# A decayed attention before two MLP blocks: the chunk of 128 with a carried state and plain float32 scores in two row halves, in place of one split at 256 and three-term scores

## The chip, the cores and the metric

One NeuronCore of a Trainium2 chip runs the whole program. The metric is the device time in microseconds (us) of one execution, the median of several. TensorE (PE) multiplies, VectorE (DVE) and ScalarE (ACT) read PSUM and do elementwise work, SyncE (SP) and GpSimd (POOL) issue the transfers (DMAs).

## What is computed

```python
batch, n_heads, seq, head_dim = (8, 8, 576, 64)
scores = scale * np.matmul(q, k.transpose(0, 1, 3, 2))
gamma = 1.0 - 2.0 ** (-5.0 - np.arange(H))
Dmat = np.where(rel >= 0, gamma[:, None, None] ** rel[None, :, :], 0.0)   # rel = query - key
x = np.matmul(scores * Dmat, v)                                 # no softmax
# tokens = batch * seq = 4608, 8 heads * 64 = 512 columns
h = np.maximum(np.maximum(x @ w1, x @ w2), x @ w3)              # 512 -> 768
x2 = h @ w_out                                                  # 768 -> 512
out = ((x2 @ u1) * (x2 @ u2)) @ u3 @ u_out                      # 512 -> 1024 -> 512
```

Since there is no softmax, a block of keys far behind its queries can be summed first into a 64x64 matrix per head (keys times decayed values, "the state"), which the decayed queries then multiply.

## The kernel before

The program has three phases. In the first, batch 0's attention runs beside the product u3 @ u_out ("wc", eight blocks, `wc_block`), whose weights and those of the first MLP arrive and are split meanwhile. In the second, a loop over b = 1 to 7, PE does the first MLP of batch b - 1 (18 `b_pair`s of two `b_unit`s each, then 8 `c_unit`s; every unit is 12 or 18 matmuls of 288 columns) and the attention of batch b in between. Last come the first MLP of batch 7 and nine tiles of the second MLP.

The MLP products are in float32r, with operands split into a high and a low part and three products (`product`, L725 to L727). Each engine executes its instructions in the order in which they are written; the semaphores between them are counted up. The order within a batch is set by `PAIR_FROM`: before head s come the b_pairs `PAIR_FROM[s]` to `PAIR_FROM[s+1]`, then on PE `values` of the earlier head pair (even s) or `sum_state` (odd s), then `scores` of head s.

For a head pair the attention is:

- `scores`, once per head (L739, L740): five blocks of the causal triangle, each as two float32r products. Rows 0 to 63 of `kstack` hold the keys' high part and rows 64 to 127 their low part, so ACT (`split_head`, L366, L367) and DVE (L548) first split keys and queries.
- DVE multiplies the scores by the decay table (`decay_head`, L566), five instructions per head.
- `sum_state` (L752): two plain float32 matmuls over the first 256 keys, of 128 columns; ACT copies the result (`read_state`, L377).
- `values` (L768, L774): the state times the decayed queries of positions 256 to 575 (128x320), and per key block and head one plain float32 matmul of 64 output rows, head 0 into PSUM partitions 0 to 63 and head 1 into 64 to 127.

A plain float32 matmul shows in the trace as two MATMUL records, each with a weight load (LDWEIGHTS, engine row PEld).

In the wc phase DVE's order matters: `split_u3(s + 1)`, which makes the low part of the next wc block's weights (u3lo), stands behind the attention work of step s. SP's queue loads every head's and pair's arrays, with waits for their buffers; POOL's queue loads u_out, u3 and the MLP weights.

Of the kernel before, what the change touches and what calls it, by code (L numbers as in the profile page):

```python
# [4 lines left out]
P = 128  # L23
# [8 lines left out]
PAIRS = HEADS // 2  # L32
# [5 lines left out]


SPLIT = 256  # L40
REST = SEQ - SPLIT
SB = SPLIT // P
KB = 5

BLOCKS = [
    (0, 0, 0, SPLIT),
    (0, 256, 3, SEQ - 3 * P),
    (0, 448, 4, SEQ - 4 * P),
    (1, 0, 1, SPLIT - P),
    (1, 128, 2, REST),  # L50
]
BANKS = 2
P_AT = [0, 256, 384, 704, 896]
P_COLS = 960
# [5 lines left out]
C_UNITS = KT * 2  # L60
# [4 lines left out]
PAIR_FROM = [0, 3, 5, 7, 9, 11, 13, 15, 18]  # L65
# [5 lines left out]

# [3 lines left out]
def build(nc, qT, kT, kP, vP, w1, w2, w3, w_out, u1, u2, u3T, u_out, decay, qdecay, vdecay, out):  # L75
# [7 lines left out]
    with ctx:  # L83
# [24 lines left out]
        qraw = at("qraw", [P, 2, SEQ], f32, o); o += 2 * SEQ * 4  # L108
        kraw = at("kraw", [P, 2, SEQ], f32, o); o += 2 * SEQ * 4
        qhi = at("qhi", [P, SEQ], f32r, o); o += SEQ * 4  # L110
        qlo = at("qlo", [P, SEQ], f32r, o); o += SEQ * 4
        kstack = at("kstack", [P, SEQ], f32r, o); o += SEQ * 4
        vals = at("vals", [P, 2, KB, P], f32, o); o += 2 * KB * P * 4
        probs = at("probs", [P, 2, P_COLS], f32, o); o += 2 * P_COLS * 4
        dec = at("dec", [P, 2, REST], f32, o); o += 2 * REST * 4
        kblk = at("kblk", [P, SB, P], f32, o); o += SB * P * 4
        vdec = at("vdec", [P, SB, P], f32, o); o += SB * P * 4
        state = at("state", [P, P], f32, o); o += P * 4
        qpair = at("qpair", [P, REST], f32, o); o += REST * 4
        qtab = at("qtab", [P, PAIRS, REST], f32, o); o += PAIRS * REST * 4  # L120
        vtab = at("vtab", [P, HEADS, SB], f32, o); o += HEADS * SB * 4
# [41 lines left out]
        ps_score, ps_state, ps_att, ps_moe = ps[0:2], ps[2], ps[4:6], ps[6:8]  # L163
# [6 lines left out]
        qk_loaded = [sem(f"qk_loaded{i}") for i in range(2)]  # L170
        dec_loaded = [sem(f"dec_loaded{i}") for i in range(2)]
        v_loaded = [sem(f"v_loaded{i}") for i in range(2)]
        split_hi = sem("split_hi")
        split_lo = sem("split_lo")
        scored = sem("scored")
        decayed = sem("decayed")
        vtab_loaded = sem("vtab_loaded")
        qtab_loaded = sem("qtab_loaded")
        k_loaded = sem("k_loaded")
        q_loaded = sem("q_loaded")  # L180
# [3 lines left out]
        state_read = sem("state_read")  # L184
# [50 lines left out]
        def _(sp):  # L235
            def load_head(b, s):
                n = HEADS * b + s
                if not (isinstance(b, int) and n < 2):
                    sp.wait_ge(split_lo, 2 * n - 2)
                for half in range(2):  # L240
                    rows = slice(DH * half, DH * half + DH)
                    sp.dma_start(kraw[rows, s % 2, :], kT[b, s, :, :]).then_inc(qk_loaded[s % 2], 16)  # L242
                for half in range(2):
                    rows = slice(DH * half, DH * half + DH)
                    sp.dma_start(qraw[rows, s % 2, :], qT[b, s, :, :]).then_inc(qk_loaded[s % 2], 16)  # L245
                if not (isinstance(b, int) and n < 2):
                    sp.wait_ge(decayed, BANKS * (n - 1))
                sp.dma_start(dec[:, s % 2, :], decay[s, :, :]).then_inc(dec_loaded[s % 2], 16)

            def load_values(b, p):  # L250
                n = PAIRS * b + p
                if isinstance(b, int) and n < 1:
                    sp.wait_ge(zeroed, 4)
                if not (isinstance(b, int) and n < 2):
                    sp.wait_ge(valued, n - 1)
                sp.dma_start(vals[:, p % 2, 0:4, :],
                             vP[b, p, 0:4 * P, :].rearrange("(n p) c -> p n c", p=P)
                             ).then_inc(v_loaded[p % 2], 16)
                sp.dma_start(vals[0:SEQ - 4 * P, p % 2, 4, :], vP[b, p, 4 * P:SEQ, :]
                             ).then_inc(v_loaded[p % 2], 16)  # L260

                if not (isinstance(b, int) and n < 1):
                    sp.wait_ge(summed, n)
                sp.dma_start(kblk[:, :, :], kP[b, p, 0:SPLIT, :].rearrange("(n p) c -> p n c", p=P)
                             ).then_inc(k_loaded, 16)

            def load_pair_queries(b, p):
                n = PAIRS * b + p
                if not (isinstance(b, int) and n < 1):
                    sp.wait_ge(valued, n)  # L270
                sp.dma_start(qpair[:, :], qT[b, 2 * p:2 * p + 2, :, SPLIT:SEQ].rearrange("h d n -> (h d) n")
                             ).then_inc(q_loaded, 16)

            def load_batch(b):
                for s in range(HEADS):
                    load_head(b, s)
                    if isinstance(b, int) and s == 0:
                        sp.dma_start(vtab[:, :, :], vdecay).then_inc(vtab_loaded, 16)
                    if isinstance(b, int) and s == 1:
                        sp.dma_start(qtab[:, :, :], qdecay).then_inc(qtab_loaded, 16)  # L280
                    if s % 2 == 0:
                        load_values(b, s // 2)
                    else:
                        load_pair_queries(b, s // 2)

            load_batch(0)
            with sp.Fori(1, BATCH) as b:
                load_batch(b)
# [55 lines left out]

# [15 lines left out]
        def _(act):  # L360
            def split_head(b, s):
                n = HEADS * b + s
                act.wait_ge(qk_loaded[s % 2], 64 * (HEADS // 2 * b + s // 2 + 1))
                if not (isinstance(b, int) and n == 0):
                    act.wait_ge(scored, BANKS * n)
                nc.scalar.copy(kstack[:, :], kraw[:, s % 2, :]).then_inc(split_hi, 1)  # L366
                nc.scalar.copy(qhi[:, :], qraw[:, s % 2, :]).then_inc(split_hi, 1)  # L367

            def read_state(b, p):

                n = PAIRS * b + p
                act.wait_ge(summed, n + 1)
                if not (isinstance(b, int) and n == 0):
                    act.wait_ge(valued, n)
                for h in range(2):
                    own = slice(h * DH, h * DH + DH)
                    nc.scalar.copy(state[own, own], ps_state[own, own]).then_inc(state_read, 1)  # L377

            def read_values(b, p):
                n = PAIRS * b + p  # L380
                act.wait_ge(valued, n + 1)
                if not (isinstance(b, int) and b == 0):
                    act.wait_ge(x_lo, n - KT + 1)
                nc.scalar.copy(xraw[:, p, 0:SPLIT], ps_att[0][:, 0:SPLIT]).then_inc(x_out, 1)
                nc.scalar.copy(xraw[:, p, SPLIT:SEQ], ps_att[1][:, 0:REST]).then_inc(x_out, 1)

# [30 lines left out]
            def batch(b):  # L417

                for s in range(HEADS):
                    split_head(b, s)  # L420
                    for i in range(PAIR_FROM[s], PAIR_FROM[s + 1]):
                        b_pair(b - 1, i)
                    if s % 2:
                        read_state(b, s // 2)
                    elif s:
                        read_values(b, s // 2 - 1)
                for c in range(4):
                    if c < 3:
                        split_x(b, c)
                    c_unit(b - 1, c)  # L430
                read_values(b, PAIRS - 1)
                split_x(b, PAIRS - 1)
                for c in range(4, C_UNITS):
                    c_unit(b - 1, c)
# [16 lines left out]
            split_head(0, 0)  # L451
# [5 lines left out]
            for s in range(HEADS):  # L457
                if s % 2:
                    read_state(0, s // 2)
                elif s:  # L460
                    read_values(0, s // 2 - 1)
                if s + 1 < HEADS:
                    split_head(0, s + 1)
# [81 lines left out]
        def _(dve):  # L545
# [4 lines left out]
            def split_head(b, s):  # L550
                n = HEADS * b + s
                dve.wait_ge(split_hi, 2 * n + 1)
                low(kstack[DH:P, :], kraw[DH:P, s % 2, :], kstack[DH:P, :]).then_inc(split_lo, 1)
                dve.wait_ge(split_hi, 2 * n + 2)
                low(qlo[:, :], qraw[:, s % 2, :], qhi[:, :]).then_inc(split_lo, 1)
# [388 lines left out]
```

## Time and profile before

| | |
|---|---|
| median of 3 runs | 1456.09 us (1454.52 to 1457.38) |
| span of the profiled execution | 1455.5 us, mean granted TensorE clock 0.998 |
| PE busy | 1427.3 us (98%) |
| weight loads (PEld) | 1273.5 us (87%) |
| DVE busy, ACT busy | 523.8 us (36%), 407.4 us (28%) |
| DMA | 117.47 MB, mean 81 GB/s |

The profiled execution's own time is its span, 0.6 us under the median. "Busy" is the union of an engine's instructions; since matmuls are pipelined and their ends modelled, PE's progress is read from the distance between starts, not from durations. The chain that ended last, followed back from the end, tells which engine set the time.

### The profile page before, as it was taken

The page shows a single profiled execution, that of the slowest core. Times are in us where ns is not written, and L with a number is a line of the kernel's source. Part 1 is how long each engine was busy: PE and PEld are TensorE (multiplying, and loading weights), DVE is VectorE, ACT ScalarE, POOL GpSimd, SP SyncE. Part 2 cuts the span into 40 slices and gives each one's busy share as a digit, 9 for nine tenths or more (in the row PEclk, how much of TensorE's full clock was granted, in tenths as well). Part 3 has the DMA queues.
Part 4 walks back from the last instruction along what each step waited for, and adds up shares of the span by engine and source line. Part 5 has one row for each costly group of instructions (what it writes and reads, how often), then busy time and mean ns, then how long its engine had stood idle before and what let it go on. Part 6 is the DMA issues. An engine that isn't in the chain of part 4 may idle for free.

```text
span 1455.5 us, 23828 instructions
## 1 busy us (share of the span) xinstructions
PE 1427.3 (98%) x8864; PEld 1273.5 (87%) x8864; DVE 523.8 (36%) x1080; ACT 407.4 (28%) x801; POOL 21.2 (1%) x40
## 2 busy tenths in 40 slices
PE   6899999999999999999999999999999999999999
PEld 4689999999999999999999998888888888888887
DVE  4665435355255354352542252121211212121211
ACT  3443223223233233233322152221222222121211
POOL 2100000000000000000000000000000000000000
PEclk9999999999999999999999999999999999999999
DMA  9954324234234243243322230101010010101000
GB/s 288 311 143 116 100 74 115 91 91 115 77 95 119 65 114 101 69 115 95 95 78 91 87 120 0 59 8 50 14 43 26 32 58 0 58 7 50 14 15 29
DMA packets 87885, 117.47 MB, mean 81 GB/s; under 512 B 9777, under 2 KB 56881, under 8 KB 87857
## 3 DMA queue, kind: packets, MB, share of 16 engines
q1 hardware_dynamic: 72688, 86.68, 20.5%
q0 software_dynamic: 4800, 18.88, 3.9%
q10 hardware_dynamic: 10368, 11.54, 2.2%
q8 instruction: 18, 0.29, 0.1%
q14 instruction: 11, 0.08, 0.0%
HBM read 96.08 MB, written 20.97 MB: 80 GB/s over the span
## 4 chain that ended last, share of the span: by engine, by line
PE 96%; DMA 2%; SPq 1%; ACT 1%; DVE 0%; issue 0%; ACTq 0%
PE ps L725 24%; PE ps L727 24%; PE ps L726 24%; PE ps L885 4%; PE ps L883 4%; PE ps L884 4%; PE ps L774 4%; PE ps L739 3%; PE ps L740 2%; DMA qraw<-qT 2%; PE ps L768 2%; PE ps L752 1%; SPq L242 0%; ACT x2st L412 0%; SPq L245 0%
## 5 line engine op out<-in xcount | busy, mean ns | idle before, releaser
L725 PE MATMUL ps<-xhi,w123hi 128*128 128x288 f32 x1152 | 340.2, 295 | 5.0 <-ACT x2st L412 3.9
L727 PE MATMUL ps<-xhi,w123lo 128*128 128x288 f32 x1152 | 339.5, 295 | 0.0
L726 PE MATMUL ps<-xlo,w123hi 128*128 128x288 f32 x1152 | 339.1, 294 | 0.0
L725 PE MATMUL ps<-yhi,uhi 128*128 128x512 f32 x576 | 224.1, 389 | 0.0
L726 PE MATMUL ps<-ylo,uhi 128*128 128x512 f32 x576 | 224.1, 389 | 0.0
L727 PE MATMUL ps<-yhi,ulo 128*128 128x512 f32 x576 | 224.1, 389 | 0.0
L725 PEld LDWEIGHTS ps<-xhi,w123hi 128*128 128x128 f32 x1152 | 216.1, 188 | 6.9 <-issue 4.8
L726 PEld LDWEIGHTS ps<-xlo,w123hi 128*128 128x128 f32 x1152 | 216.2, 188 | 0.0
L727 PEld LDWEIGHTS ps<-xhi,w123lo 128*128 128x128 f32 x1152 | 216.1, 188 | 0.0
L698 DVE TENSOR_TENSOR gprod<-ps,acopy 128x512 f32<-128x512 f32 x72 | 49.8, 691 | 393.1 <-PE ps L727 393.1
L727 PEld LDWEIGHTS ps<-yhi,ulo 128*128 128x128 f32 x576 | 108.1, 188 | 22.5
L726 PEld LDWEIGHTS ps<-ylo,uhi 128*128 128x128 f32 x576 | 108.1, 188 | 22.4
L725 PEld LDWEIGHTS ps<-yhi,uhi 128*128 128x128 f32 x576 | 108.1, 188 | 22.4
L725 PE MATMUL ps<-hhi,wouthi 128*128 128x288 f32 x384 | 113.8, 296 | 0.0
L726 PE MATMUL ps<-hlo,wouthi 128*128 128x288 f32 x384 | 113.1, 295 | 0.0
L727 PE MATMUL ps<-hhi,woutlo 128*128 128x288 f32 x384 | 113.1, 294 | 0.0
L884 PE MATMUL ps<-wclo,ghi 128*128 128x512 f32 x288 | 112.0, 389 | 0.0
L883 PE MATMUL ps<-wchi,ghi 128*128 128x512 f32 x288 | 112.0, 389 | 0.0
L885 PE MATMUL ps<-wchi,glo 128*128 128x512 f32 x288 | 112.0, 389 | 0.0
L566 DVE TENSOR_TENSOR probs<-ps,dec 128x256 f32<-128x256 f32 (+4 forms) x320 | 89.9, 344 | 61.3 <-PE ps L740 60.9
L406 ACT CAST hhi<-hmax 128x288 fp32r<-128x288 f32 x96 | 41.6, 433 | 224.5 <-DVE hmax L614 224.5
L519 ACT CAST ghi<-gprod 128x512 fp32r<-128x512 f32 x72 | 44.7, 620 | 213.3 <-DVE gprod L698 213.3
(70 smaller groups left out, 1699.3 us busy)
## 6 DMA issues: line engine op xcount, KB each, us to landing
kraw<-kT SPq DMA_DIRECT2D x128, 144.0 KB, 2.8
qraw<-qT SPq DMA_DIRECT2D x128, 144.0 KB, 2.9
dec<-decay SPq DMA_DIRECT2D x64, 160.0 KB, 2.7
x2T<-x2st ACTq DMA_DIRECT2D x64, 144.0 KB, 1.8
yraw<-x2T SPq DMA_DIRECT2D x9, 1024.0 KB, 5.3
out<-ost SPq DMA_DIRECT2D x36, 256.0 KB, 2.0
vals<-vP SPq DMA_DIRECT2D x32, 256.0 KB, 2.8
qpair<-qT SPq DMA_DIRECT2D x32, 160.0 KB, 2.2
```

The lines of the kernel that those rows point to most:

```text
L406: nc.scalar.copy(hhi[:, f, cols], hmax[:, hf, :]).then_inc(h_hi, 1)
L519: nc.scalar.copy(ghi[:, f, :], gprod[:, f % 2, :]).then_inc(g_hi, 1)
L566: op = nc.vector.tensor_tensor(probs[0:nk, s % 2, P_AT[kb]:P_AT[kb] + nq], ps_score[bank][0:nk, at_col:at_col + nq], dec[0:nk, s % 2, 0:nq ...
L698: nc.vector.tensor_tensor(gprod[:, f % 2, :], ps_b[f % 2][:, :], acopy[:, f % 2, :], ALU.mult).then_inc(g_made, 1)
L725: nc.tensor.matmul(dst, shi, mhi, start=(i == 0), stop=False)
L726: nc.tensor.matmul(dst, shi, mlo, start=False, stop=False)
L727: last = nc.tensor.matmul(dst, slo, mhi, start=False, stop=(i == len(pairs) - 1))
L739: nc.tensor.matmul(dst, keys, qhi[:, kb * P:kb * P + nq], start=True, stop=False)
L774: last = nc.tensor.matmul(ps_att[bank][own, kb * P - begin:end - begin], vals[:, p % 2, kb, own], probs[:, h, P_AT[kb]:P_AT[kb] + nq], sta ...
L883: nc.tensor.matmul(dst, ghi[:, k, tok], wchi[:, k, :], start=(k == 0), stop=False)
L884: nc.tensor.matmul(dst, ghi[:, k, tok], wclo[:, k, :], start=False, stop=False)
L885: last = nc.tensor.matmul(dst, glo[:, k, tok], wchi[:, k, :], start=False, stop=(k == FT2 - 1))
```

## The change

The state is now carried over four chunks of 128 keys (`NC = 4`, the last 64 positions are `TAIL`), so that scores are needed only inside a chunk. All of the attention is in plain float32; keys and queries are no longer split. Queries and keys of one head pair come in one transfer (`kq`, 1280 columns, with a block diagonal copy of the tail queries), values and keys by tokens in another (`vk`, 1152 columns); the decay tables stay in SBUF.

```
-PAIR_FROM = [0, 3, 5, 7, 9, 11, 13, 15, 18]
+STEP_AT = [0, 3, 9, 12, 18]
...
+            def load_pair(b, p):
+                n = PAIRS * b + p
                 if not (isinstance(b, int) and n < 2):
                     sp.wait_ge(valued, n - 1)
+                sp.dma_start(kqs[:, p % 2, :], kq[b, p, :, :]).then_inc(kq_loaded[p % 2], 16)
+                if isinstance(b, int) and n == 0:
+                    sp.dma_start(dec[:, :, :], decay).then_inc(tabs_loaded, 16)
+                    sp.dma_start(vtab[:, :, :], vdecay).then_inc(tabs_loaded, 16)
+                sp.dma_start(vks[:, p % 2, :], vk[b, p, :, :]).then_inc(vk_loaded[p % 2], 16)
+                if isinstance(b, int) and n == 0:
+                    sp.dma_start(qtab[:, :, :], qdecay).then_inc(tabs_loaded, 16)
...
             def decay_values(b, p):
+                dve.wait_ge(vk_loaded[p % 2], 16 * (PAIRS // 2 * b + p // 2 + 1))
                 if isinstance(b, int) and n == 0:
+                    dve.wait_ge(tabs_loaded, 48)
                 else:
                     dve.wait_ge(summed, n)
+                nc.vector.tensor_tensor(
+                    vdec[:, :, :], vks[:, p % 2, 0:NC * CH].rearrange("p (n c) -> p n c", c=P),
+                    vtab[:, p, :].unsqueeze(1).broadcast_to([P, NC, P]), ALU.mult).then_inc(v_decayed, 1)
...
+            def make_state(b, p):
+                n = PAIRS * b + p
+                dve.wait_ge(summed, n + 1)
+                for c in range(NC):
+                    for h in range(2):
+                        own = slice(h * DH, h * DH + DH)
+                        new = ps_state[own, c * DH:(c + 1) * DH]
+                        if c == 0:
+                            nc.vector.tensor_copy(state[own, c, own], new).then_inc(state_made, 1)
+                        else:
+                            dve.wait_ge(state_made, 2 * NC * n + 2 * (c - 1) + h + 1)
+                            nc.vector.scalar_tensor_tensor(
+                                state[own, c, own], state[own, c - 1, own], CHUNK_DECAY[2 * p + h], new,
+                                ALU.mult, ALU.add).then_inc(state_made, 1)
...
             def sum_state(b, p):
+                for c in range(NC):
+                    for h in range(2):
+                        own = slice(h * DH, h * DH + DH)
+                        at_ = (NC + 1 + c) * CH + h * DH
+                        last = nc.tensor.matmul(ps_state[own, c * DH:(c + 1) * DH],
+                                                vks[:, p % 2, at_:at_ + DH], vdec[:, c, own],
+                                                start=(c == 0), stop=(c == NC - 1), skip_group_check=True)
...
+            def scores(b, p):
+                for c in range(NC):
+                    cols = slice(c * CH, (c + 1) * CH)
+                    for h in range(2):
+                        own = slice(h * DH, h * DH + DH)
+                        last = nc.tensor.matmul(ps_score[h][:, cols], kqs[own, p % 2, cols],
+                                                kqs[own, p % 2, SEQ + c * CH:SEQ + (c + 1) * CH],
+                                                start=(c == 0), stop=(c == NC - 1), skip_group_check=True)
+                nc.tensor.matmul(ps_tail[0:TAIL, 0:CH], kqs[:, p % 2, NC * CH:SEQ], kqs[:, p % 2, 2 * SEQ:KQ_COLS],
+                                 start=True, stop=True).then_inc(scored, 1)
```

`values` becomes four matmuls of a carried state with the decayed queries `qdec` and, for each of the five chunks and each head, one matmul of its values with its decayed scores. The ACT work `split_head` and `read_state` is gone.

In the loop over b, the steps j = 0 to 4 each come behind the b_pairs `STEP_AT[j-1]` to `STEP_AT[j]`; a step is `values(j-1)`, `sum_state(j)`, `scores(j)` on PE and `decay_values`, `decay_queries`, `make_state`, `decay_scores` on DVE. At j = 0 no b_pair stands ahead, and the last `values` comes ahead of all c_units.

On PE, inside the loop, the rows of a step with values, before (there a `sum_state` and a second set of scores stand two b_pairs away):

```order
L774 MATMUL ps<-probs,vals 64x256 [waits x_out,v_loaded0]
L774 MATMUL ps<-probs,vals 64x256
L774 MATMUL ps<-probs,vals 64x128 x2
L766 REGISTER_ALU
L768 MATMUL ps<-qpair,state 128x320 [waits q_decayed,state_read]
L774 MATMUL ps<-probs,vals 64x320 x2
L774 MATMUL ps<-probs,vals 64x192 x2
L774 MATMUL ps<-probs,vals 64x64 x2
```

and of the change, where `vks` holds values and keys by tokens and `kqs` keys and queries:

```order
L667 MATMUL ps<-qdec,state 128x128 [waits x_out]
L667 MATMUL ps<-qdec,state 128x128 x2
L667 MATMUL ps<-qdec,state 128x64
L669 REGISTER_ALU
L676 MATMUL ps<-probs,vks 64x128 [waits decayed]
L676 MATMUL ps<-probs,vks 64x128 x7
L676 MATMUL ps<-probs,vks 64x64 x2
L629 REGISTER_ALU
L636 MATMUL ps<-vdec,vks 64x64 [waits state_made,v_decayed]
L636 MATMUL ps<-vdec,vks 64x64 x7
L643 ISA
L650 MATMUL ps<-kqs 128x128 [waits decayed,kq_loaded0]
```

The state sum now follows the values at once and waits there for DVE's `v_decayed`; behind it come seven more score matmuls and the tail's (L655, 64x128).

On DVE, in the wc phase behind the second wc block, the change has these rows; u3lo of the next block (row L442) stands last:

```order
L461 TENSOR_TENSOR qdec<-kqs,qtab 128x384 [waits valued,kq_loaded1]
L465 TENSOR_TENSOR qdec<-kqs,qtab 128x64
L476 COPY state<-ps 64x64 [waits summed]
L476 COPY state<-ps 64x64
L479 SCALAR_TENSOR_TENSOR state<-state,ps 64x64 [waits state_made] x6
L487 TENSOR_TENSOR probs<-ps,dec 128x512 [waits scored] x2
L492 TENSOR_TENSOR probs<-ps,dec 64x2x64 [waits scored]
L451 TENSOR_TENSOR vdec<-vks,vtab 128x512 [waits summed,vk_loaded0]
L442 TENSOR_TENSOR u3lo_78<-u3raw_80,u3hi_76 128x1024 [waits u3_hi]
```

Before, the same stretch of the wc phase, where the decayed values wait for smaller transfers that were asked for earlier:

```order
L548 TENSOR_TENSOR kstack<-kraw,kstack 64x576 [waits split_hi]
L548 TENSOR_TENSOR qlo<-qraw,qhi 128x576 [waits split_hi]
L581 TENSOR_TENSOR vdec<-vals,vtab 128x2x64 [waits summed,v_loaded0]
L581 TENSOR_TENSOR vdec<-vals,vtab 128x2x64
L548 TENSOR_TENSOR u3lo_83<-u3raw_85,u3hi_81 128x1024 [waits u3_hi]
```

So u3lo has moved behind a wait for a whole `vk` transfer, which SP issues only when the values two pairs earlier are done (`valued`).

## Rows read from the trace of the kernel before

**Rows 1.** The page: span, and the chain that ended last.

```profile
span 1455.5 us, 23828 instructions
PE 96%; DMA 2%; SPq 1%; ACT 1%; DVE 0%; issue 0%; ACTq 0%
```

**Rows 2.** All waits of PE: waiting line, awaited line, total us, times, longest.

```profile
PE ps L739 <- DVE qlo L548: 13.3, 1, 13.3
PE ps L752 <- DVE vdec L581: 6.8, 2, 6.2
PE ps L725 <- ACT x2st L412: 3.9, 7, 0.6
```

**Rows 3.** One batch of the loop, busy us and instructions by engine.

```profile
217.13:316.54 99.41, 98.84 (x763) 93.51 (x764) 45.01 (x109) 30.01 (x68) 0.00 (x0) 1.00 0.33 96
```

**Rows 4.** PE's timeline, loop, state sum and scores: start, us, engine, line.

```profile
209.03 0.61 PE L752 MATMUL ps<-vdec,kblk 128*128 128x128 f32 x4
209.40 0.36 PE L739 MATMUL ps<-qhi,kstack 128*128 128x256 f32 x1
...
210.61 0.30 PE L725 MATMUL ps<-xhi,w123hi 128*128 128x288 f32 x1
```

**Rows 5.** PE's timeline, loop: end of a b_pair; then values and scores.

```profile
201.55 0.27 PE L739 MATMUL ps<-qhi,kstack 128*128 128x256 f32 x1
...
216.84 0.29 PE L727 MATMUL ps<-xhi,w123lo 128*128 128x288 f32 x1
217.06 0.87 PE L774 MATMUL ps<-probs,vals 128*64 128x256 f32 x8
217.86 0.81 PE L768 MATMUL ps<-qpair,state 128*128 128x320 f32 x2
218.60 1.20 PE L774 MATMUL ps<-probs,vals 128*64 128x320 f32 x12
219.73 0.38 PE L739 MATMUL ps<-qhi,kstack 128*128 128x256 f32 x1
...
220.96 0.30 PE L725 MATMUL ps<-xhi,w123hi 128*128 128x288 f32 x1
```

**Rows 6.** The same timeline, its first 0.12 us alone.

```profile
217.06 0.44 PE L774 MATMUL ps<-probs,vals 128*64 128x256 f32 x2
```

**Rows 7.** DVE's timeline behind the b_pair that ended at 201.55.

```profile
201.83 0.46 DVE L614 TENSOR_TENSOR hmax<-ps,hmax 128x288 f32<-128x288 f32 x1 [1.14 <-PE ps L727]
202.21 1.04 DVE L548 TENSOR_TENSOR hlo<-hmax,hhi 128x288 fp32r<-128x288 f32 x2
203.16 0.49 DVE L581 TENSOR_TENSOR vdec<-vals,vtab 128x128 f32<-128x128 f32 x2
```

**Rows 8.** Groups of DVE instructions: busy us, mean ns of one.

```profile
L698 DVE TENSOR_TENSOR gprod<-ps,acopy 128x512 f32<-128x512 f32 x72 | 49.8, 691 | 393.1 <-PE ps L727 393.1
L566 DVE TENSOR_TENSOR probs<-ps,dec 64x64 f32<-64x64 f32 x64 | 13.2, 206 | 0.0
```

**Rows 9.** DMA queues from 4 to 16 us (q0 POOL's, q1 SP's), and one issue group of all.

```profile
q0 software_dynamic: 809, 2.92, 73.2%
q1 hardware_dynamic: 1281, 1.02, 30.8%
...
yraw<-x2T SPq DMA_DIRECT2D x9, 1024.0 KB, 5.3
```

**Rows 10.** PE's timeline, wc phase, and the chain's piece ahead of the stall at 63.

```profile
15.56 0.79 PE L725 MATMUL ps<-uohi,u3hi 128*128 128x512 f32 x1
...
63.04 1.23 PE L752 MATMUL ps<-vdec,kblk 128*128 128x128 f32 x4 [6.23 <-DVE vdec L581]
...
88.44 0.87 PE L774 MATMUL ps<-probs,vals 128*64 128x256 f32 x8
...
93.68 0.40 PE L725 MATMUL ps<-xhi,w123hi 128*128 128x288 f32 x1 [1.07 <-DVE xlo L548]
...
42.85 17.46 DMA qraw<-qT
```

More of the change, by code:

```diff
@@ L35 @@
 NT = TOKENS // TILE
[L40 to L54, printed above, removed]
+CH = 128
+NC = SEQ // CH
+TAIL = SEQ - NC * CH
+LATER = SEQ - CH
+KQ_COLS = 2 * SEQ + CH
+GAMMA = [1.0 - 2.0 ** (-5.0 - h) for h in range(HEADS)]
+CHUNK_DECAY = [g ** CH for g in GAMMA]
+VK_COLS = (NC + 1) * CH + NC * CH
 SLOTS = 4
@@ L235, in _ @@
         def _(sp):
[L236 to L248, printed above, removed]
@@ L267, in load_pair_queries @@
[L267 to L284, printed above, removed]
@@ L287, in _ @@
+            for p in range(PAIRS):
+                load_pair(0, p)
             with sp.Fori(1, BATCH) as b:
-                load_batch(b)
+                for p in range(PAIRS):
+                    load_pair(b, p)
             def load_y(t):
@@ L360, in _ @@
         def _(act):
[L361 to L377, printed above, removed]
             def read_values(b, p):
@@ L747, in sum_state @@
                 pe.wait_ge(v_decayed, n + 1)
-                pe.wait_ge(k_loaded, 16 * n + 16)
                 if not (isinstance(b, int) and n == 0):
-                    pe.wait_ge(state_read, 2 * n)
-                for i in range(SB):
-                    last = nc.tensor.matmul(ps_state[:, 0:P], kblk[:, i, :], vdec[:, i, :],
-                                            start=(i == 0), stop=(i == SB - 1))
-                last.then_inc(summed, 1)
+                    pe.wait_ge(state_made, 2 * NC * n)
@@ new lines, in values @@
+                for c in range(1, NC + 1):
+                    w = min(CH, SEQ - c * CH)
+                    dst = ps_att[0][:, c * CH:c * CH + w] if c < NC else ps_att[1][:, 0:w]
+                    nc.tensor.matmul(dst, state[:, c - 1, :], qdec[:, (c - 1) * CH:(c - 1) * CH + w],
+                                     start=(c == 1 or c == NC), stop=False, skip_group_check=True)
+                pe.wait_ge(decayed, 3 * (n + 1))
+                for c in range(NC + 1):
+                    w = min(CH, SEQ - c * CH)
+                    for h in range(2):
+                        own = slice(h * DH, h * DH + DH)
+                        dst = ps_att[0][own, c * CH:c * CH + w] if c < NC else ps_att[1][own, 0:w]
+                        at_ = c * CH + h * DH
+                        last = nc.tensor.matmul(dst, vks[0:w, p % 2, at_:at_ + DH],
+                                                probs[0:w, h, c * CH:c * CH + w],
+                                                start=False, stop=(c >= NC - 1), skip_group_check=True)
@@ L830, in _ @@
             for s in range(HEADS):
-                if s % 2:
+                if s % 2 == 0:
+                    if s:
+                        values(0, s // 2 - 1)
                     sum_state(0, s // 2)
-                elif s:
-                    values(0, s // 2 - 1)
-                scores(0, s)
+                    scores(0, s // 2)
                 wc_block(s)
@@ L841, in _ @@
             with pe.Fori(1, BATCH) as b:
-                for s in range(HEADS):
-                    for i in range(PAIR_FROM[s], PAIR_FROM[s + 1]):
+                for j in range(PAIRS + 1):
+                    for i in range(STEP_AT[j - 1] if j else 0, STEP_AT[j]):
                         b_pair(b - 1, i)
-                    if s % 2:
-                        sum_state(b, s // 2)
-                    elif s:
-                        values(b, s // 2 - 1)
-                    scores(b, s)
-                for c in range(4):
-                    c_unit(b - 1, c)
-                values(b, PAIRS - 1)
-                for c in range(4, C_UNITS):
+                    if j:
+                        values(b, j - 1)
+                    if j < PAIRS:
+                        sum_state(b, j)
+                        scores(b, j)
+                for c in range(C_UNITS):
                     c_unit(b - 1, c)
@@ L931 @@
         "u_out": inputs["moe2_w_out"],
[L932 removed]
+        "decay": decay.transpose(1, 0, 2).astype(np.float32),
         "qdecay": qdecay.astype(np.float32),
```

241 lines of the change are left out of this document (85 added, 156 removed).

## The prediction

> **What bounds the kernel now.** I read the chain first: 96% of the span is PE, 2% a DMA [rows 1]. PE's waits come next, since only they are not its own work: 13.3 us before its first matmul, 6.2 us in the wc phase, and seven waits of about 0.57 us on an ACT copy of `x2st` (L412), one per batch, where the first b_unit needs the PSUM of the last c_unit [rows 2]. One batch of the loop lasts 99.41 us at a granted clock of 1.00, and PE is busy 98.84 us of it [rows 3]; DVE has 45 us of work there and ACT 30. So in the loop every us of PE's attention counts, once for each of 7 batches, while DVE's and ACT's work is free as long as nobody waits for it. The second MLP behind the loop is not touched. Only the wc phase, the first 91 us, has other limits: transfers and what DVE does ahead of each u3lo.
>
> **What PE spends on a head pair now.** The state sum and one set of scores take 209.03 to 210.61, 1.58 us [rows 4]. The values with the other set take from the end of the last product to 220.96. That product started at 216.84 and costs 0.13, so it ends at 216.97, and the piece is 3.99 us [rows 5]. Together 5.57 us a pair. Check: (99.41 - 0.57 - 4 x 5.57) / 576 products is 0.133 us for one of 288 columns, which is how far the products stand apart.
>
> **What a plain float32 matmul costs.** The first stretch of L774 (8 records, two heads and two passes, 256 + 128 columns) lasts 217.06 to 217.86, 0.80 us; the second (12 records, 320 + 192 + 64 columns) 218.60 to 219.73, 1.13 us [rows 5]. The difference, 0.33 us for 192 more columns, is 1.72 ns per column for both passes; 0.80 - 384 x 0.00172 leaves 0.14 us per stretch. Of this 0.09 lies between stretches whose matmuls use the array in different shapes (216.97 to 217.06 shows it too), and 0.05 is the first weight load of 64 columns. L768 takes 0.74 for 320 columns: 0.55 + 0.19, so a first load of 128 columns is 0.10 to 0.11. Four passes of 128 columns with 128-column weights take 209.03 to 209.40 and a little more: 0.11 a pass, weights and columns alike [rows 4]. The two heads cost the time of one: in the first 0.12 us two records have started already, long before one of 0.43 us can be over [rows 6]. They stand in two halves of the columns.
>
> **PE's new work per pair.** `values`: four state matmuls, 8 passes x 0.11 = 0.88 (the 64-column one pays its weight load). Change of shape and load 0.14; both heads' 512 columns 0.88; their 64-column tail 0.11. State sum, same shape: 4 x 64 columns x 1.72 ns = 0.44. Scores: change 0.09, load 0.11, 8 passes x 0.11 = 0.88, **if** the two heads' row halves run together as the column halves do. Tail: change 0.09 + load 0.05 + 128 columns 0.22; back to products 0.20. Sum 4.09, I take 4.1. Below: 3.9, if the tail's full-height matmul needs no change back. Above: 4.37, if the 64-row tail of the values is a shape of its own (twice 0.14).
>
> The trace has no row halves, so this cost is bounded: together 0.88 as computed, one after the other 1.76. The nearest row is the column pair [rows 6], and each head has its own rows and its own PSUM bank, so I take together. The Trainium skill, "TensorE: Matmul & The Clock Gate", Part 3, says that matmuls in different row groups start some 4 ns apart, and would give the same 4.1 us. The same page, Part 2, says that a weight load's time goes by its columns, whatever its rows; if the halves' loads also queued, that would be 0.22 a pass and 4.97 us a pair. No row here shows either. "TensorEngine Tiling (Array Packing)", Key Properties, says that changing the tiling mode drains TensorE; the 0.09 us gap agrees, and it speaks against this change, which has one or two such changes more per pair.
>
> **New wait.** `sum_state(j)` comes straight behind `values(j-1)` and needs `v_decayed`. DVE can start `decay_values` only behind the b_pair's last hlo: 203.16 against PE's end of the b_pair at 201.55, 1.61 us later [rows 5, 7]. The 128x512 multiply is the size of `gprod`, 0.69 [rows 8], so `v_decayed` comes at 2.36 after the b_pair. PE's values are done at 2.01 to 2.15. PE waits 0.3 us, at j = 1, 2, 3; at j = 0 DVE is long free. Queued behind it are scores and the next b_pair. Further on DVE: `decay_queries` 0.75, eight 64x64 state instructions at 0.206 = 1.65, scores 2 x 0.69 + 0.27 [rows 8]: done at about 6.6. PE is then in the first b_pair (evacuated by ACT), and DVE is next needed when the third unit ends, at 4.4 + 3.2 + 1.6 = 9.2. That cover of 2.6 us hides the carried state. The copies that ACT loses were hidden. One removed wait: at j = 0 PE does state sum and scores (about 2 us) between the last c_unit and the first b_unit, so the 0.57 us for `x2st` go, but for the last batch, which stands outside the loop.
>
> **Transfers.** A pair needs 128 x (1280 + 1152) x 4 B = 1.245 MB. 1.05 MB land in 5.3 us [rows 9], so this takes 6.5. In the loop the shortest stretch from `valued` to need is three b_pairs and a step, 13 us: hidden.
>
> **Loop.** Before 4 x 5.57 + 0.57 = 22.85; after 4 x 4.1 + 3 x 0.3 = 17.3. 5.55 x 7 - 0.57 = **38.3 us** less.
>
> **The wc phase.** PE's first matmul is at 13.3, wc block 0 starts at 15.56, the last `values` at 88.44, and the first b_unit goes on at 93.68, when the last xlo is there [rows 2, 10]. Now `decay_values(0, 0)` needs 2.29 MB from SP's queue (kq, vk, three tables). The queues moved 3.94 MB in 12 us, 0.33 MB/us, only 0.085 of it SP's, with small packets (1.02 MB in 1281) against POOL's (2.92 MB in 809) [rows 9]. SP's new packets are as large as POOL's, so I give it half: 2.29 / 0.16 + 2.1 = 16.5, about 17 us. Then vdec, two 1.2 us splits (1.08 ns a column by [rows 8]) : block 0 at 20.2, 4.6 later than before. Block 1 waits for DVE's queue (uolo, qdec, state, scores, vdec, u3lo): 29.7. From there PE needs 5.45 for a block and 4.1 for a step, a wc block pair being 15 us. At blocks 3 and 5, u3lo stands behind `decay_values`, which waits for a vk that SP asks for only at `valued`: 37.3 + 1.245 / 0.18 + 1.5 = 46, + 0.7 + 1.2 = 48, PE ready at 44.8: 3.1 us lost, and again 3.1 at block 5, which starts at 66. Before, PE had its 6.23 us stall at 63.04. Blocks 5 to 7 and the steps end at 86.8, values at 88.8, last xlo at 92. Against 93.68: **1.6 us** less, uncertain by 5 either way.
>
> **Sum.** 1455.5 - 38.3 - 1.6 = 1415.6 by the span; the median of the runs is 0.6 above it: **1416 us**.
>
> **Rivals.** (1) The row halves run one after the other, or their loads do: + 0.88 x 28 in the loop and + 3.5 in the wc phase: 1444 (1430 to 1456). For it: no row half in this trace. Against: rows 6. (2) Slower than before: the vk transfers of the wc phase come so late that u3lo stalls PE for more than the gain. `qraw` once took 17.46 us to land behind the same queues [rows 10]. The loads have some 7 us of cover, so the two of them (pairs 2 and 3) must each take 7 + 20 = 27 us before the 40 us are eaten; at 17.5 they cost 10 each, 13.7 over my count in all, 1430. At 30 us each, which needs half the slowest rate seen, 1461. (3) No change: the chain is not PE's attention, since something that I count as hidden (state chain on DVE, 2.6 us of cover) takes it all back: the eight state instructions would have to cost 0.2 + (2.6 + 1.4) / 8 = 0.7 us each instead of 0.206. About 1456.
>
> **Numbers.** Forecast case 0.74 (1402 to 1435: 3.9 without waits and 6 less in the wc phase below, 4.37 with 0.5 us waits and 5 more above), rival 1 0.19, rival 2 0.03, rival 3 0.04. The range that holds 8 in 10 goes from 1402 up into rival 1: 1442. Of rival 1 nearly all is still over 0.2% faster, which is about what a measurement of this kernel can tell from no change: faster 0.92, same 0.04, slower 0.04.
>
> **What would show it.** A batch of the loop near 94 us. From the first L667 to the next product about 4.1 us, plus 0.3 of wait on L451 at j = 1 to 3. In the scores (L650) 8 passes for both heads 0.11 apart; if 0.22, rival 1. L412 releases PE once instead of seven times. Waits of PE for u3lo near 27, 45 and 62 us. If the loop comes out at 94 and the total does not, the wc phase was wrong; if changes of shape cost more than 0.09, the step is over 4.4 us.

## The result, and the profile after

The changed kernel takes 1459.91 us (median of 20 runs, 1455.02 to 1463.3), the kernel before 1455.94 beside it (20 runs): a ratio of 1.0028, 95% interval 1.0021 to 1.0035. It is 0.28% slower. The prediction of 1416 us, with a range to 1442 and a chance of 0.92 on faster, was wrong. The profiled execution has a span of 1460.2 us, against 1455.5 [rows 1].

The page of the changed kernel: span, busy rows, instruction fetches, and the chain that ended last.

```profile
span 1460.2 us, 23628 instructions
PE 1406.2 (96%) x9376; PEld 1267.9 (87%) x9376; DVE 459.6 (31%) x981; ACT 316.7 (22%) x609; POOL 21.2 (1%) x40
q8 instruction: 73, 1.20, 0.3%
PE 91%; DVE 3%; DMA 2%; issue 2%; ACT 1%; POOL 0%; DVEq 0%; SPq 0%; ACTq 0%; POOLq 0%
```

PE has 21 us less to do than before, and the program is longer all the same: time in which PE does nothing, or works at a lower clock, took its place. All waits of PE (waiting line, awaited line, total us, times, longest) show two rows that the kernel before has not [rows 2]:

```profile
PE ps L636 <- DVE vdec L451: 20.7, 2, 15.4
PE ps L622 <- DVE u3lo L442: 10.6, 3, 4.2
PE ps L650 <- issue: 9.6, 6, 1.7
PE ps L636 <- issue: 7.9, 6, 1.5
PE ps L622 <- ACT x2st L318: 0.5, 1, 0.5
```

"Issue" means that PE waited for nothing that the profile shows. It comes twice in each of the six passes behind a jump back of the loop (L742 in the changed kernel). Here is such a place in PE's timeline (start, us, engine, line): the jump follows the last product of a c_unit.

```profile
296.12 0.29 PE L624 MATMUL ps<-hhi,woutlo 128*128 128x288 f32 x1
297.96 0.69 PE L636 MATMUL ps<-vdec,vks 128*64 128x64 f32 x16 [1.54 <-issue]
298.57 0.94 PE L650 MATMUL ps<-kqs 64*128 64x128 f32 x12
300.85 0.49 PE L650 MATMUL ps<-kqs 64*128 64x128 f32 x4 [1.34 <-issue]
301.27 0.43 PE L655 MATMUL ps<-kqs 128*64 128x128 f32 x2
301.63 0.51 PE L622 MATMUL ps<-xhi,w123hi 128*128 128x288 f32 x1
301.94 0.45 PE L623 MATMUL ps<-xlo,w123hi 128*128 128x288 f32 x1
302.18 0.45 PE L624 MATMUL ps<-xhi,w123lo 128*128 128x288 f32 x1
...
305.06 0.36 PE L624 MATMUL ps<-xhi,w123lo 128*128 128x288 f32 x1
305.25 0.29 PE L622 MATMUL ps<-xhi,w123hi 128*128 128x288 f32 x1
305.38 0.29 PE L623 MATMUL ps<-xlo,w123hi 128*128 128x288 f32 x1
```

PE stands still for 1.54 us ahead of the state sum and again for 1.34 us in the middle of the scores, between two matmuls of one group on data that is all there. After that the products stand 0.24 us apart until 305.06 and 0.13 us again afterwards: the granted clock is at the lower of its two levels (1.2 instead of 2.4 GHz) for 3.4 us, and for 6.8 us in the first of the six.

The jump itself has a record, in PE's sequencer (count, shortest/median/longest in ns, first and last start in us). The branch at the end of PE's loop, in the changed kernel and in the kernel before:

```profile
L742 PEldq COMPARE_BRANCH  x7: 83/3396/3723, 193.5 to 790.1; - x7
L841 PEldq COMPARE_BRANCH  x7: 76/208/234, 188.9 to 785.3; - x7
```

The last of the seven doesn't jump. The six that do take 3.3 to 3.7 us in the changed kernel and 0.21 to 0.23 before.

The queues of one batch of the changed kernel, 296.12 to 395.39, have something that the kernel before has not (packets, MB, share):

```profile
q1 hardware_dynamic: 1152, 4.98, 14.0%
q10 hardware_dynamic: 1155, 1.18, 3.4%
q8 instruction: 9, 0.15, 0.6%
```

Nine packets of 16 KB are instructions. In the kernel before the same stretch (290.46 to 389.87) has no row of q8, and the whole program 18 packets. One batch of the changed kernel (busy us and instructions of PE, PEld, DVE, ACT, POOL, then granted clock, DMA share, GB/s) lasts about as long as before [rows 3], with PE idle for 3.1 us of it:

```profile
296.12:395.39 99.27, 96.16 (x827) 92.87 (x825) 37.00 (x96) 18.58 (x44) 0.00 (x0) 0.98 0.18 64
```

The six batches between the last c_units of the loop's first pass and of its last take 596.5 us, before 596.4: the loop gained nothing. The first of these ends stands at 195.7 us, before at 191.1, so the start lost 4.6 us, and that is the whole difference of the spans.

Inside the loop, away from the jump, the step itself:

```profile
312.67 0.30 PE L624 MATMUL ps<-xhi,w123lo 128*128 128x288 f32 x1
312.81 1.00 PE L667 MATMUL ps<-qdec,state 128*128 128x128 f32 x8
313.74 1.35 PE L676 MATMUL ps<-probs,vks 128*64 128x128 f32 x20
315.17 0.69 PE L636 MATMUL ps<-vdec,vks 128*64 128x64 f32 x16
315.78 1.16 PE L650 MATMUL ps<-kqs 64*128 64x128 f32 x16
316.87 0.43 PE L655 MATMUL ps<-kqs 128*64 128x128 f32 x2
317.24 0.40 PE L622 MATMUL ps<-xhi,w123hi 128*128 128x288 f32 x1
```

From the last product's end (312.80) to the next one's start is 4.44 us; 4.1 + 0.3 were forecast. That first product then takes 0.23 us instead of 0.13 (317.24 to 317.47), so that the step costs 4.54. The 16 score records of both heads take 1.09 us with the change of shape.

### The profile page after: what moved, and what is told of

It is laid out like the page before. It is cut to its first block, busy times and chain, and to the rows that moved or that the text cites. A ratio compares the mean times of both kernels' runs of the same rounds, so it can differ in the third digit from the quotient of the medians.

```text
span 1460.2 us, 23628 instructions
## 1 busy us (share of the span) xinstructions
PE 1406.2 (96%) x9376; PEld 1267.9 (87%) x9376; DVE 459.6 (31%) x981; ACT 316.7 (22%) x609; POOL 21.2 (1%) x40
## 4 chain that ended last, share of the span: by engine, by line
PE 91%; DVE 3%; DMA 2%; issue 2%; ACT 1%; POOL 0%; DVEq 0%; SPq 0%; ACTq 0%; POOLq 0%
PE ps L622 24%; PE ps L624 24%; PE ps L623 24%; PE ps L782 4%; PE ps L783 4%; PE ps L781 4%; PE ps L650 2%; PE ps L636 1%; DMA vks<-vk 1%; DVE vdec L451 1%; DMA uoraw<-u_out 1%; PE ps L676 1%; PE ps L655 1%; DVE hmax L517 1%; ACT hhi L312 1%
## 5 line engine op out<-in xcount | busy, mean ns | idle before, releaser
L622 PE MATMUL ps<-xhi,w123hi 128*128 128x288 f32 x1152 | 346.3, 301 | 0.5 <-ACT x2st L318 0.5
L624 PE MATMUL ps<-xhi,w123lo 128*128 128x288 f32 x1152 | 343.1, 298 | 0.0
L623 PE MATMUL ps<-xlo,w123hi 128*128 128x288 f32 x1152 | 342.8, 298 | 0.0
L622 PEld LDWEIGHTS ps<-xhi,w123hi 128*128 128x128 f32 x1152 | 219.8, 191 | 6.4 <-issue 5.7
L623 PEld LDWEIGHTS ps<-xlo,w123hi 128*128 128x128 f32 x1152 | 220.1, 191 | 0.0
L624 PEld LDWEIGHTS ps<-xhi,w123lo 128*128 128x128 f32 x1152 | 219.6, 191 | 0.0
L512 DVE TENSOR_TENSOR hmax<-ps,first 128x288 f32<-128x288 f32 x96 | 44.0, 458 | 236.5 <-PE ps L624 236.5
```

Source lines behind the costliest of these rows:

```text
L512: nc.vector.tensor_tensor(hmax[:, hf, :], ps_moe[hf][:, 0:HALF], first[:, hf, :], ALU.max).then_inc(dve_evac, 1)
L622: nc.tensor.matmul(dst, shi, mhi, start=(i == 0), stop=False)
L623: nc.tensor.matmul(dst, shi, mlo, start=False, stop=False)
L624: last = nc.tensor.matmul(dst, slo, mhi, start=False, stop=(i == len(pairs) - 1))
```

## The experiments

The theory after this first look: **PE's loop no longer stays in its instruction store, so each jump back waits for a fetch, twice, and the clock falls behind it.** Two things could lie behind it: the loop is longer (1732 PE instructions a pass instead of 1621, from one branch record to the next) or it starts elsewhere (at PE instruction 903 of the built program instead of 784). The rival: state and score matmuls at the start of a pass wait for something else, a buffer or DVE, that the profile calls issue.

**1. PE's loop written out** (the changed kernel, 7 copies of the body on PE alone).

```
-            with pe.Fori(1, BATCH) as b:
+            for b in range(1, BATCH):
```

> The changed kernel with PE's loop over the batches written out, same work in the same order, so that PE never jumps back. Theory (instruction fetch): the pauses of 1.5 and 1.9 us behind each of the 6 jumps back and the half clock of 3.4 us behind them come from instructions that have to be fetched anew; they go, 6 x 4.7 = 28 us, about 1432 us, and the granted clock stays full in the loop. Rival A (low activity of the row and column halves makes the clock fall): pauses may go, the half clock stays, 3.0 x 6 = 18 us, 1442. Rival B (the pauses are waits for semaphores or data): no change, 1460.

Measured: 1431.28 us, ratio 0.9831 (0.9814 to 0.9847). A batch:

```profile
290.91:385.43 94.52, 94.30 (x827) 91.26 (x825) 36.98 (x96) 18.58 (x44) 0.00 (x0) 1.00 0.19 66
```

No issue gaps and no lower clock in the loop. Yet the program fetches 0.95 MB of instructions in 58 packets: a fetch that runs ahead of PE in a straight line costs nothing; one that a jump asks for does. The theory holds, and the six passes are worth 596.5 - 567.1 = 29 us, 4.9 each (4.7 in most, 5.9 in the first).

**2 and 3. Length or place.** Empty instructions ahead of PE's first one move the loop without making it longer: 135 of them, then 60.

```
+            for _ in range(60):
+                pe.nop(nofuse=True).then_inc(filler, 1)
             pe.wait_ge(zeroed, 1)
```

> The changed kernel with 135 instructions without work ahead of PE's first matmul, where PE idles anyway. By the built program the loop's 1732 PE instructions then lie in 7 pages of 256 and not in 8. Theory (instruction fetch, the loop is kept if it lies in 7 pages): no instruction fetches inside the loop after its first pass, pauses and half clock gone, about 1432 us. Rival C (the jump itself costs the pauses, wherever the loop lies): 1460, pauses unchanged. Rival B: 1460.

> As the last, but with 60 such instructions: the loop still lies in 8 pages. Theory: as the changed kernel, 1460 us, fetches in every pass. If instructions without work helped by themselves, it would lie between.

With 135: 1448.41 us, ratio 0.9945 (0.9928 to 0.9961), still 74 fetch packets and branch records of 3.5 to 4.2 us, but one pause a pass instead of two, and half clock behind only two of six. The total hides some of that gain, since these empty instructions hold PE's first matmul back from 15.4 to 21.6 us. With 60: 1431.22 us, ratio 0.9838 (0.9821 to 0.9854), 19 packets, none of them between 179 and 764 us, and branch records of 0.21 to 0.23 us. A batch, with 60:

```profile
290.91:385.43 94.52, 94.30 (x826) 91.27 (x826) 36.98 (x97) 18.58 (x44) 0.00 (x0) 1.00 0.18 65
```

I had expected it the other way round: the border that I had guessed was wrong. That place decides, and not length alone, was right. The same loop of 1732 instructions is kept when it starts at 963, and fetched anew at 903 and at 1038. Run 3 still has the jump and has no pause, so the jump as such costs none of this.

**4 and 5. The kernel before, moved** by 180 and by 119 empty instructions; the second starts its loop at 903, where the changed kernel has it.

> The kernel before with 180 instructions without work ahead of PE's first matmul: its loop of 1621 PE instructions lies in 8 pages and no longer in 7. Theory: fetches in every pass, and a pause at each jump back, which the slower use of instructions by the b_pairs (two per 0.133 us) partly hides: 1 to 2 us at each of 6 jumps and perhaps the half clock, 1462 to 1475 us. Rivals B and C: no change, 1456.

> The kernel before with 119 instructions without work ahead of PE's first matmul, so that its loop starts at the same PE instruction (903) as the changed kernel's. Read from the batch periods of the trace (99.41 us in the kernel before), not from the total, which the 119 instructions lengthen at 0.16 us each (some 5 us here). Theory (the loop must lie in 7 pages, whose borders by the first four runs are between instruction 903 and 963, mod 256): 1621 instructions from there need 8 pages, so fetches in every pass and a longer period: a pause of about 1.5 us at the jump, partly in the 0.73 us gap that is there already: 100.2 to 101 us, and 102 if the clock falls. Rival (the changed kernel's loop is refetched because it is longer or has other instructions, wherever it starts): no fetches in the loop, 99.4.

With 180: 1470.79 us, ratio 1.0103 (1.0086 to 1.012), no fetch in the loop, branch records of 0.21 to 0.23 us, batches of 99.41. The expectation was missed with the same guessed border; the 15 us are the empty instructions themselves, 0.16 us each, which hold PE's first matmul back to 28.4 us. With 119: 1465.68 us, ratio 1.0067 (1.0047 to 1.0087), 73 packets and branch records of 3.3 to 3.7 us as in the changed kernel, and batches of 99.97 to 100.37, for the most part just under the 100.2 to 101 expected:

```profile
294.57:394.54 99.97, 98.83 (x762) 93.50 (x761) 45.02 (x108) 30.12 (x68) 0.00 (x0) 1.00 0.33 97
```

So the kernel before can be made to fetch too, but it pays only 0.6 to 1.0 us a pass: there the pause of 1.1 to 1.5 us covers the 0.57 us wait for x2st, and products of 288 columns stand at the loop's head. In the changed kernel the second pause comes behind 56 matmuls and loads (16 and 12 MATMUL records, with their loads), which last 1.3 us; in products 56 of them last 28 x 0.133 = 3.7 us, there is no second pause, and the clock stays at 1.00.

All six placements (903, 963 and 1038 for the changed loop, 784, 903 and 964 for the one before) fit one rule: instructions lie in blocks of 256 (16 KB, one packet), a border is at 1 to 60 instructions behind number 903 and then every 256, and a loop that touches 7 blocks is kept, one that touches 8 is fetched anew. The changed loop is kept when it starts in the first 60 of a block (963, and again in run 11), the one before in the first 171 (784, 964, but not 903). The second pause, behind 56 loads and matmuls and four register instructions, so 60 behind 903, falls on the border that this gives; in run 2 the next border is over 120 instructions away, and there is one pause. The size of a block can be estimated from runs 1 and 3: 39 packets more for 6 x 1732 instructions more, 266 to a packet. The rule is inferred from where fetches and pauses fall, not read off, and six placements leave room for another one.

The Trainium skill, "Runtime: NRT & Kernel Launch", "Instruction fetch mechanics", says that a taken branch whose target is outside the current window of two pages forces a fetch before execution goes on, and gives a store of 2048 instructions for PE in blocks of 256. Blocks of some 266 instructions, and the pause at the jump, are what these traces show. 2048 instructions are 8 blocks, while by the rule above a loop that touches 8 is not kept. The window of two pages is not what they show: by two pages the kernel before would fetch at each pass, and it has no packet in the loop. The page also says that sequential fetches are mostly hidden, and runs 1 and 10 agree (58 and 54 packets, no pause).

**6. The first step behind b_pairs** (so that products stand at the head of the loop), and shorter stretches between.

```
-STEP_AT = [0, 3, 9, 12, 18]
+STEP_AT = [3, 6, 9, 12, 18]
```

> The changed kernel with the steps at b_pairs 3, 6, 9, 12, 18, so that three b_pairs and not the first step stand behind the jump back; PE's instructions and their place are the same in number, so the fetches stay. If the pauses come from the state sum and the scores using up instructions faster than they are fetched, the second pause (1.9 us) goes, the first (1.5) stays, and the clock stays full: 2 + 1.6 of 4.7 us at six jumps, less 0.5 for a wait on vdec at j = 0: about 1441 us. If the pause belongs to the step wherever it stands, 1460.

Measured: 1459.09 us, ratio 1.0019 (1.001 to 1.0029). The second pause is gone, as in run 5, but a wait for `vdec` came in its place. The first stays, 1.1 to 1.6 us at six jumps; four of the six stand in the row of x2st, which comes late there too. All waits of PE over 0.5 us:

```profile
PE ps L636 <- DVE vdec L451: 30.9, 8, 15.0
PE ps L622 <- DVE u3lo L442: 9.9, 3, 3.4
PE ps L622 <- ACT x2st L318: 5.4, 5, 1.3
PE ps L622 <- issue: 3.2, 2, 1.6
```

A step 0 behind a b_pair has no values ahead of its state sum, so it bears DVE's whole delay: 30.9 - 15.0 is 15.9 us in seven waits, 2.3 each. The order written in the change avoids that wait. Behind four of the seven the clock falls too (batches of 98.35 to 99.97 us). The expectation was missed, since it had this wait at 0.5 us.

**7 to 9. The start.** There the changed kernel waits for u3lo three times and once more, 5.3 us at 99.56, for the decayed values of the loop's first step. PE's timeline:

```profile
15.45 1.12 PE L636 MATMUL ps<-vdec,vks 128*64 128x64 f32 x16 [15.45 <-DVE vdec L451]
...
27.97 0.50 PE L622 MATMUL ps<-uohi,u3hi 128*128 128x512 f32 x1 [3.37 <-DVE u3lo L442]
...
49.41 0.79 PE L622 MATMUL ps<-uohi,u3hi 128*128 128x512 f32 x1 [4.21 <-DVE u3lo L442]
...
69.49 0.67 PE L622 MATMUL ps<-uohi,u3hi 128*128 128x512 f32 x1 [3.00 <-DVE u3lo L442]
```

DVE's timeline ahead of 99.56 has the reason for the fourth: the multiply that PE needs stands last, behind four splits of x and one of weights.

```profile
92.95 2.10 DVE L442 TENSOR_TENSOR xlo<-xraw,xhi 128x576 fp32r<-128x576 f32 x3 [1.95 <-ACT xhi L300]
96.39 0.76 DVE L442 TENSOR_TENSOR xlo<-xraw,xhi 128x576 fp32r<-128x576 f32 x1 [1.34 <-ACT xhi L300]
97.06 1.75 DVE L442 TENSOR_TENSOR woutlo<-woutraw,wouthi 128x1536 fp32r<-128x1536 f32 x1
98.73 0.68 DVE L451 TENSOR_TENSOR vdec<-vks,vtab 128x512 f32<-128x512 f32 x1
```

With each of the four the clock goes to its lower level, 3.4 us three times and then 6.8 us (the clock of the window is the 0.50 behind the five engines):

```profile
97.00:103.83 6.83, 4.28 (x36) 3.61 (x37) 5.88 (x15) 0.00 (x0) 0.00 (x0) 0.50 0.44 176
```

Run 7 changes DVE's order: u3lo ahead of the decayed values, and the decayed values of the loop's first step ahead of the splits of x. For the latter DVE's loop had to be written out too, and the last split of weights moved up as well. Run 8 does all this and writes PE's loop out. Run 9 writes PE's loop out and moves u3lo only; DVE's loop stays a loop in it.

```
             for s in range(HEADS):
+                if s == 0:
+                    split_u3(1)
...
-                    if s // 2 + 1 < PAIRS:
-                        decay_values(0, s // 2 + 1)
-                if s + 1 < WC_UNITS:
+                if 0 < s and s + 1 < WC_UNITS:
                     split_u3(s + 1)
+                if s % 2 == 0 and s // 2 + 1 < PAIRS:
+                    decay_values(0, s // 2 + 1)
...
+            decay_values(1, 0)
             for p in range(PAIRS):
                 split_x(0, p)
...
-            with dve.Fori(1, BATCH) as b:
+            for b in range(1, BATCH):
...
-                        decay_values(b, j)
+                        if b > 1 or j:
+                            decay_values(b, j)
```

> The changed kernel with another order on DVE in the wc phase: u3lo of the next block ahead of the decayed values of the next pair (and ahead of all for block 1), the last weight split and the decayed values of batch 1, pair 0, ahead of the splits of x; DVE's loop is written out for this, PE's is not. The waits of PE for u3lo (3.4, 4.2, 3.0 us) and for vdec at the first step of the loop (5.3), with the half clock behind them, should go or shrink: 4.2 + 3.0 + 5.3 + 4 = 10 to 16 us, about 1446. If the transfers of weights are what holds the wc phase, 3 us or less, 1457.

> Both mends together: PE's loop written out and DVE's order in the wc phase. The two places don't touch, so the gains add: 1431 less 10 to 16 us, 1415 to 1421 (my forecast for the change was 1416).

> The changed kernel with PE's loop written out, and on DVE in the wc phase only the order of u3lo: split_u3(1) first at s = 0, split_u3(s + 1) ahead of decay_values of the next pair. decay_values(1, 0) keeps its place behind split_x. Theory (the start loses to two things of its own, each with a stretch of half clock behind it): the three waits of PE for u3lo (3.4, 4.2 and 3.0 us in the changed kernel) and the half clock behind them go, together 14 to 16 us, and the wait of 5.3 us at the first step of the loop with its 6.8 us of half clock stays, 7 to 9 us: 1415 to 1418 us. Rival (it is decay_values(1, 0) alone that gave the 23 us): 1429 to 1431. Other rival (u3lo alone gave all of it): 1408.

| run | us | ratio, 95% interval | end of the loop's first pass, us |
|---|---|---|---|
| changed kernel | 1459.91 | 1.0028 (1.0021 to 1.0035) | 195.7 |
| 7: order alone | 1437.3 | 0.9871 (0.9854 to 0.9887) | 173.6 |
| 1: loop written out alone | 1431.28 | 0.9831 (0.9814 to 0.9847) | 196.4 |
| 9: written out, u3lo moved | 1416.14 | 0.9733 (0.9706 to 0.9761) | 178.7 |
| 8: written out, whole order | 1407.89 | 0.9671 (0.9655 to 0.9687) | 172.9 |

The two causes add up: the order gives 22.6 us with PE's loop as in the change and 23.4 with it written out. Of the latter u3lo is 15.1 and the rest 8.3. Some 1.6 of the 8.3 are not the first step's but come with DVE's written-out loop: a batch takes 94.23 to 94.27 us in runs 8 and 11 and 94.50 to 94.53 in runs 1, 3 and 9, because three state sums a batch start 0.09 us earlier. That leaves 6.7 for the first step. Both parts are more than the waits that they remove (10.9 and 5.2 in run 1), since the lower clock that comes with the waits goes too. I had expected 14 us for the whole order in run 7 and 1415 to 1421 in run 8, and so had priced the lower clock too low; run 9 came as expected. In run 8 PE waits for next to nothing in the start but its first operands:

```profile
PE ps L638 <- DVE vdec L451: 14.5, 1, 14.5
PE ps L624 <- ACT x2st L318: 0.5, 1, 0.5
PE ps L624 <- ACT first L309: 0.2, 1, 0.2
```

Run 7 also prices the pieces of the pause. Its loop has three kinds of passes, with 6.8, 0 and 3.4 us at the lower clock:

```profile
272.53:373.17 100.64, 97.44 (x827) 93.92 (x825) 36.74 (x96) 18.59 (x44) 0.00 (x0) 0.97 0.18 63
373.17:470.43 97.26, 94.57 (x826) 91.33 (x825) 36.74 (x96) 18.59 (x44) 0.00 (x0) 1.00 0.18 65
470.43:569.45 99.02, 96.09 (x826) 92.58 (x825) 36.74 (x96) 18.59 (x44) 0.00 (x0) 0.98 0.18 64
```

Run 8 has 94.27. So the two pauses cost 3.0 us, and each 3.4 us of lower clock some 1.7 more (0.2 to 0.3 of which are slightly longer pauses in those passes). What decides whether the clock falls behind a pause stays open: in run 2 single pauses of 1.98 us were followed by it twice, those of 1.3 to 1.7 not; in run 6 waits of 2.28 us were followed by it four times and three times not.

**10. Control: PE's loop of the kernel before written out.**

> The kernel before with PE's loop over b written out for 7 batches, nothing else. Theory (the kernel before keeps its loop in PE's instruction store, so there is nothing to gain): 1455 to 1457 us, a batch stays 99.4 us, and PE's instructions are fetched throughout with no pause. Rival (a jump back costs something in the kernel before too, such as part of the 0.86 us at each c_unit's end that is put down to x2st): up to 7 x 0.8 less, 1450.

Measured: 1456.37 us, ratio 1.0001 (0.9989 to 1.0014), batches of 99.35. Writing the loop out is worth nothing where it was kept, as expected.

**11. The loop kept, the order changed, 60 empty instructions.**

> The changed kernel with DVE's order in the start as in the best one, PE's loop kept, and 60 empty instructions ahead of PE's first one. Theory (the placement of the loop decides alone, and the 60 instructions run while PE waits for vdec): 1407 to 1409 us, a batch of 94.3 us, no fetch of PE's instructions inside the loop. Rival (the loop is fetched again at each pass, as where DVE's order alone was changed): 1437.

Measured: 1408.83 us, ratio 0.9678 (0.965 to 0.9706), batches of 94.23 to 94.25, 19 packets, as expected. It does what run 8 does with a seventh of the loop's PE code; the 60 empty instructions cost next to nothing here, since PE waits for vdec until 15.06.

## Why the prediction was wrong

- **PE's work per pair and the wait for `v_decayed`: right, if a little low.** The batch without fetches is 94.23 to 94.53 us, "a batch of the loop near 94 us". The sum gives 99.41 - 5.55 = 93.86; with DVE's loop as in the change it is 0.66 more (94.52): 0.15 in each of three steps, where the state sum alone is 0.17 over its term, and the rest in the fourth, which is split between the two ends of a batch. The state matmuls took 0.93 (forecast 0.88), values with the wait 1.43 (1.13 + 0.3), the state sum 0.61 (0.44), scores with the change of shape 1.09 (1.08), the tail 0.37 (0.36); coming back to products cost 0.10, in the first product, where 0.20 were taken. By this the step is 4.54, against 4.39. DVE's vdec was there at 315.11, 2.3 us after the b_pair, as worked out. The changes of shape were taken at 0.09 each, and the pieces that hold them came out as forecast.
- **Row halves (rival 1): refuted.** 16 records in 1.09 us leave no room for one head after the other, or for loads that queue, which needed 1.76.
- **The x2st wait goes but for one: right.** L412 became L318, with one wait.
- **State chain on DVE (rival 3): refuted.** Neither the changed kernel nor run 8 has a wait of PE for it in the loop.
- **"So in the loop every us of PE's attention counts, once for each of 7 batches": the failed step.** The sum built on it, "5.55 x 7 - 0.57 = 38.3 us less", took the matmuls removed as time removed and put the jump back of the loop at nothing, without a reason. The loop as changed is fetched anew at each of six jumps, which costs 4.9 us each, 29 us in all (runs 1 and 3). Six batches were to gain 6 x 5.55 = 33 us; without the fetches they gain 29, and the other 4 are the 0.66 a batch above. That the six batches take 596.5 us against 596.4 before is chance: 29 us of less work and 29 us of fetches have nothing to do with each other.
- **The start: wrong by 11.7 us.** By the forecast the first pass ends at 191.1 - 1.6 - 5.5 = 184.0; it ended at 195.7. The waits for u3lo near 27, 45 and 62 came (27.97, 49.41, 69.49), and block 0 at 18.9 (forecast 20.2). Two things were left out. The clock behind each wait: the last values end at 94.3 instead of 88.8. And the first step of the loop, where "at j = 0 DVE is long free" is wrong in the first pass: its `decay_values` stands on DVE behind the splits of x: 5.3 us, and half clock with that. Runs 7 to 9 show both. The order of a moved step had been read on PE and not on DVE.
- **Late transfers (rival 2)**: not the cause. The two vk transfers that u3lo stood behind took 9.7 and 8.4 us, not 17.5, and the waits of 4.2 and 3.0 us are near the 3.1 forecast for each; with the same transfers, run 8 has no wait for u3lo. By the prediction's own count (1430 at 17.5 us each) transfers of 30 us, 23 over their cover, give 1416 + 2 x 23 - 2 x 3.1 = 1456 and not 1461: the rival as priced meant no change.

The rival that came true stood in no list: that the change moves code, and code has a place.

## What to carry to other kernels

Count the instructions of a loop's body on the busiest engine, and look at the instruction queue in the profile and at the record of the loop's branch: packets inside the loop, a branch of 3 us instead of 0.2, and gaps put down to issue right behind it mean that the loop is not kept. Then an edit ahead of the loop can move the time too, here by 2% with 60 empty instructions. Compare two versions with the loop written out before judging either. When a step is moved to a loop's start, follow its producers on the other engines too; and price a stall of PE with the stretch of lower clock behind it.

## What the runs showed of the hardware

- A loop of 1732 PE instructions is kept or fetched anew depending on where it starts, with 4.9 us a pass between the two; one of 1621 likewise, with 0.6 to 1.0.
- The branch record tells the two apart at once: 0.21 to 0.24 us where the loop was kept, 3.3 to 4.2 us where it was fetched anew, in the nine kernels here whose PE loop is not written out.
- Fetches in a straight line were hidden everywhere, 54 to 58 packets; after a jump PE stood for 1.1 to 2.0 us, and again for 1.3 to 1.8 us where, by the rule above, the next block began only 56 short matmul records and loads later.
- Two row halves of 64 run side by side in plain float32: 16 records in 1.09 us with a change of shape and a first load; without these two, by an estimate, 128 columns of both heads, both passes, in 0.22 us.
- An empty instruction that raises a semaphore costs PE 0.16 us.
